# Attention and two mixture layers on one core: operands laid out as the engines read them, and three attention blocks in other slots

## The reference, cut to what matters

```python
scores = scale * np.matmul(q, k.transpose(0, 1, 3, 2))
mask = (rel >= 0) & (rel < 64)            # rel = query position - key position
scores = np.where(mask, scores, -1000000000.0)
attn = softmax(scores)                    # exp(s - max) / (sum + 1e-9)
x = matmul(attn, v)                       # -> (2304, 512), heads side by side
```

## Time and profile before

| | us |
|---|---|
| median of three runs | 1084.02 (1082.53 to 1084.6) |
| the profiled execution, its own time | 1084.5 |
| its span, first to last instruction | 1082.8 |
| TensorE busy | 1047.7 (97%) |
| start of `gate_val(0)`, from the span's start | 40.81 |

### The profile page before, as it was taken

One profiled execution on the slowest core, in us unless ns is written; L12 is line 12 of the kernel. 1 busy time (PEld: TensorE's weight loads), 2 busy tenths in 40 slices (PEclk: granted clock), 3 DMA queues, 4 the chain that ended last, 5 costly groups with the idle time before them and its releaser, 6 DMA issues. The chain is left out here.

```text
span 1082.8 us, 19239 instructions
## 1 busy us (share of the span) xinstructions
PE 1047.7 (97%) x7599; PEld 957.4 (88%) x7599; DVE 404.4 (37%) x1131; ACT 396.5 (37%) x959; POOL 233.9 (22%) x225
## 2 busy tenths in 40 slices
PE   6799999999999999999999999999999999999994
PEld 5699999999999999999999989889898989898993
DVE  4364334343343434333245534423242434342410
ACT  5344343343434334343324532433332433333310
POOL 2266003012021211202012041330403031211211
PEclk8699999999999999999999999999999999999997
DMA  7565214222122222211212350562536354453302
GB/s 160 129 185 118 49 30 108 54 70 60 47 62 50 69 50 79 54 36 31 78 41 89 117 143 30 156 139 85 137 97 152 102 136 117 102 151 90 66 12 38
DMA packets 121211, 95.31 MB, mean 88 GB/s; under 512 B 83232, under 2 KB 95776, under 8 KB 121120
## 3 DMA queue, kind: packets, MB, share of 16 engines
q1 hardware_dynamic: 108032, 66.48, 21.6%
q0 software_dynamic: 12032, 27.31, 12.1%
q10 hardware_dynamic: 1056, 0.26, 0.1%
HBM read 72.35 MB, written 21.68 MB: 87 GB/s over the span
## 5 line engine op out<-in xcount | busy, mean ns | idle before, releaser
L784 PEld LDWEIGHTS bank<-xr,wr 128*128 128x128 f32 x2592 | 326.5, 191 | 9.3 <-issue 0.5
L784 PE MATMUL bank<-xr,wr 128*128 128x256 f32 x2592 | 329.4, 284 | 0.0
L865 PE MATMUL bank<-wr 128*128 128x256 f32 (+1 forms) x1536 | 229.8, 309 | 0.6 <-DVE xr L1439 0.3
L865 PEld LDWEIGHTS bank<-wr 128*128 128x128 f32 x1536 | 226.1, 190 | 1.4 <-DVE wr L1439 0.6
L801 PE MATMUL bank<-wr,hr 128*128 128x512 f32 x648 | 176.4, 407 | 0.0
L1066 ACT ACTIVATE arena<-bank 128x256 f32<-128x256 f32 x108 | 41.3, 383 | 282.6 <-PE bank L784 282.6
L1333 DVE SCALAR_TENSOR_TENSOR arena<-arena,bank 128x256 f32<-128x256 f32 x108 | 45.5, 421 | 259.4 <-ACT arena L1066 252.2
L880 PE MATMUL bank<-wr 128*128 128x512 f32 x576 | 136.3, 393 | 0.0
L801 PEld LDWEIGHTS bank<-wr,hr 128*128 128x128 f32 x648 | 113.7, 189 | 22.9 <-issue 2.8
L880 PEld LDWEIGHTS bank<-wr 128*128 128x128 f32 x576 | 106.6, 188 | 21.5
L602 POOL DMA_INDIRECT out<-arena,tab x34 | 53.4, 1572 | 283.8 <-ACT arena L1145 275.4
(11 more groups left out here) (127 smaller groups left out, 846.6 us busy)
## 6 DMA issues: line engine op xcount, KB each, us to landing
arena<-moe_w SPq DMA_DIRECT2D x64, 512.0 KB, 3.8
arena<-v SPq DMA_DIRECT2D x70, 128.0 KB, 3.2
out<-zeros POOLq DMA_DIRECT2D x20, 256.0 KB, 2.7
arena<-k SPq DMA_DIRECT2D x36, 128.0 KB, 3.1
x_rows<-arena SPq DMA_DIRECT2D x9, 512.0 KB, 2.8
arena<-q SPq DMA_DIRECT2D x34, 128.0 KB, 3.2
arena<-moe_w_gate SPq DMA_DIRECT2D x12, 256.0 KB, 3.3
arena<-moe_w_val SPq DMA_DIRECT2D x12, 256.0 KB, 4.0
```

The lines of the kernel that those rows point to most:

```text
L784: mm = pe.matmul(o, gv_w[:, f, w, kk], xr[:, g % 2, x, kk], start=(m + kk + n == 0), stop=(kk == KC - 1 and n == 2), skip_group_check=True)
L865: mm = pe.matmul(ps_h[u % 2][:, 0:n], w1_r[e % 2][:, a, kk, f * P:(f + 1) * P], xT[p][:, b, kk], start=(kk + x == 0), stop=(kk == KC - 1 a ...
```

## The change

In `kernel`, numpy rearranges four inputs before the launch. q and k become arrays of 18 pairs x 128 x 2 blocks x 4 x 64: 128 partitions hold the head dimension of two heads, so that they land in `qT` and `kT` as the matmul reads them, 2 KB for each partition. v becomes rows of 512 floats. w_gate and w_val become one array `gv`, 4 KB for each partition and chunk. `turn_k`, `turn_q`, `copy_k` and `copy_q` go, with the waits on `q_copied`. `qT` gets two buffers. The factor -1/8 moves into the `scale` of the instruction in `mask_max` (`scale=-SCALE`), and the mask's fill becomes negative. The loads of k and q of pair t now stand in slot 6t-21 and wait for the scores that read the buffer. The scores of block 5 move from the opening into slot 0, turn_p of block 4 into slot 1, and each step of blocks 4 to 7 gets a slot from a table; blocks 8 and on stay in their slots. `split_high` and `split_low` of chunks 0 and 1 stand later in the opening's order.

```diff
+    S_LATE = {5: 0, 6: 2, 7: 4}
+    E_LATE = {5: 1, 6: 3, 7: 5}
+    SUM_LATE = {4: 0, 5: 2, 6: 4, 7: 6}
+    P_LATE = {4: 1, 5: 3, 6: 5, 7: 7}
+    PV_LATE = {4: 2, 5: 4, 6: 6, 7: 8}
+    X_LATE = {4: 3, 5: 5, 6: 7, 7: 10}
+    MIXED_LATE = {3: 3, 7: 4}
+    V_LATE = 5
...
+        def stage(s, offset, late):
+            for n, at in late.items():
+                if at == s:
+                    return n
+            n, off = divmod(s - offset, 3)
+            return n if off == 0 and max(late) < n < NB else None
...
             def load_k(t):
-                if t:
-                    sp.wait_ge(k_turned, t)
-                for half in range(2):
-                    sp.dma_start(k_nat[half * WIN:(half + 1) * WIN].rearrange("p (h d) -> p h d", h=H),
-                                 of_block(k, 2 * t + half)).then_inc(k_in, 16)
+                if t >= 2:
+                    sp.wait_ge(s_done, 2 * t - 1)
+                sp.dma_start(kT[:, t % 2:t % 2 + 3:2], k[t]).then_inc(k_in[t % 2], 16)
             def load_q(t):
-                sp.wait_ge(q_turned, t)
-                for half in range(2):
-                    sp.dma_start(q_nat[half * WIN:(half + 1) * WIN].rearrange("p (h d) -> p h d", h=H),
-                                 of_block(q, 2 * t + half)).then_inc(q_in, 16)
+                if t >= 2:
+                    sp.wait_ge(s_done, 2 * t - 2)
+                sp.dma_start(qT[:, t % 2], q[t]).then_inc(q_in[t % 2], 16)
...
-                for m, src in enumerate((gate_d, val_d)):
-                    sp.dma_start(gv_raw[:, f % 2, m], src[f]).then_inc(gv_in[f % 2], 16)
+                sp.dma_start(gv_raw[:, f % 2].rearrange("p m k n -> p (m k n)"), gv[f]).then_inc(gv_in[f % 2], 16)
...
-            load_k(0)
+            sp.dma_start(kT[:, 0], k[0, :, 0]).then_inc(k_first, 16)
+            sp.dma_start(kT[:, 2], k[0, :, 1]).then_inc(k_in[0], 16)
             load_mixed(0)
             load_v(0)
+            load_k(1)
             load_weights(0)
-            load_k(1)
-            load_q(1)
             load_weights(1)
+            load_k(2)
+            load_q(2)
             load_mixed(1)
-            load_k(2)
             load_v(1)
-            load_q(2)
             load_weights(2)
             load_mixed(2)
+            load_v(2)
             load_k(3)
+            load_q(3)
             load_weights(3)
-            load_v(2)
-            load_q(3)
-            load_k(4)
...
-            turn_k(0)
-            turn_q(0)
             scores(0)
             scores(1)
-            turn_k(1)
-            turn_q(1)
             turn_p(0)
             scores(2)
             values(0)
             turn_p(1)
             scores(3)
             values(1)
             turn_p(2)
-            turn_k(2)
             values(2)
-            turn_q(2)
             turn_p(3)
             values(3)
             scores(4)
-            turn_k(3)
-            turn_q(3)
-            scores(5)
             for s in range(LAST):
                 g, f = divmod(s, FC)
                 if 0 <= s < LAST:
                     gate_val(g, f)
-                if s == 0:
-                    turn_p(OPEN)
-                    values(OPEN)
-                if (n := at_slot(s, 3, -18, NB)) is not None:
+                if (n := stage(s, -18, S_LATE)) is not None:
                     scores(n)
-                if (n := at_slot(s, 3, -14, NB)) is not None:
+                if (n := stage(s, -14, P_LATE)) is not None:
                     turn_p(n)
-                if (n := at_slot(s, 3, -13, NB)) is not None:
+                if (n := stage(s, -13, PV_LATE)) is not None:
                     values(n)
                 if g >= 2 and f == 0:
                     rank_rows(g - 2)
-                if (t := at_slot(s, 6, -20, TT)) is not None:
-                    turn_k(t)
-                if (t := at_slot(s, 6, -19, TT)) is not None:
-                    turn_q(t)
...
-            act.dma_start(q_nat[half * WIN:(half + 1) * WIN].rearrange("p (h d) -> p h d", h=H),
-                              of_block(q, half)).then_inc(q_in, 16)
+            act.dma_start(qT[:, 0, 0], q[0, :, 0]).then_inc(q_first, 16)
+            act.dma_start(qT[:, 0, 1], q[0, :, 1]).then_inc(q_in[0], 16)
+            act.dma_start(qT[:, 1], q[1]).then_inc(q_in[1], 16)
```

More of the change, by code:

```diff
@@ L14, with attention_two_moe_program @@
 P = 128
[L17 to L26, removed]
+def attention_two_moe_program(nc, q, k, v, gv, w_out, r_gate, r_noise, noise, w1, w2, out):
+    TT, P_, _, GP, WIN = q.shape
+    TOK, DM = v.shape
+    HD = P_ // 2
+    FC = gv.shape[0]
+    DF = FC * P
+    NB = 2 * TT
+    B = 4
+    BLOCKS = NB // B
     SCALE = float(HD) ** -0.5
@@ L29, in attention_two_moe_program @@
     KC = DM // P
-    FC = DF // P
     GT = 2 * P
@@ L62, in attention_two_moe_program @@
     assert (CH * TOK + AHEAD * HT - 2 * TILES * P) // P < MORE
-    assert (HD, WIN, GP, KC, FC) == (64, 64, 4, 4, 12) and S == BLOCKS * WIN and NB == 4 * GROUPS == 2 * TT
+    assert (HD, WIN, GP, KC, FC) == (64, 64, 4, 4, 12) and TOK == NB * WIN and NB == 4 * GROUPS == B * BLOCKS
     assert NW == FC * DM
@@ L217, in attention_two_moe_program @@
         out_t = out.rearrange("(t p) d -> t p d", p=P)
-        k_in = sem("k_in")
-        q_in = sem("q_in")
+        k_first = sem("k_first")
+        q_first = sem("q_first")
+        k_in = [sem(f"k_in{u}") for u in range(2)]
+        q_in = [sem(f"q_in{u}") for u in range(2)]
         v_in = sem("v_in")
         m_in = sem("m_in")
[L222 to L225, removed]
         s_done = sem("s_done")
@@ L397, in load_v @@
                     sp.wait_ge(pv_done, 2 * t)
-                for half in range(2):
-                    sp.dma_start(v_nat[half * WIN:(half + 1) * WIN].rearrange("p (h d) -> p h d", h=H),
-                                 of_block(v, 2 * t + half)).then_inc(v_in, 16)
+                sp.dma_start(v_nat[:], v[t * P:(t + 1) * P]).then_inc(v_in, 16)
             def load_mixed(t):
@@ L606, in _ @@
             split_out(1)
-            scale(OPEN)
             for s in range(LAST):
-                if (n := at_slot(s, 3, -15, NB)) is not None:
+                if (n := stage(s, -15, SUM_LATE)) is not None:
                     scale(n)
@@ L679, in _ @@
         def _(pe):
[L680 to L704, removed]
             def scores(n):
                 c0, c1 = keys(n)
-                pe.wait_ge(k_copied, n // 2 + 1)
-                pe.wait_ge(q_copied, n // 2 + 1)
+                if n == 0:
+                    pe.wait_ge(k_first, 16)
+                    pe.wait_ge(q_first, 16)
+                else:
+                    pe.wait_ge(k_in[n // 2 % 2], 16 * (n // 4 + 1))
+                    pe.wait_ge(q_in[n // 2 % 2], 16 * (n // 4 + 1))
                 if n > OPEN:
@@ L725, in scores @@
                             if starts(n):
-                                window = kT[rows, c, place(n)]
+                                window = kT[rows, place(n), c * WIN:(c + 1) * WIN]
                             else:
                                 even, odd = sorted((place(n - 1), place(n)))
-                                window = kT[rows, c, even:odd + 1:odd - even]
-                            mm = pe.matmul(ps_sc(n)[h][j * WIN:(j + 1) * WIN, i * P + c0:i * P + c1], qT[rows, c, n % 2], window,
+                                window = kT[rows, even:odd + 1:odd - even, c * WIN:(c + 1) * WIN]
+                            mm = pe.matmul(ps_sc(n)[h][j * WIN:(j + 1) * WIN, i * P + c0:i * P + c1], qT[rows, n // 2 % 2, n % 2, c * WIN:(c + 1) * WIN], window,
                                            start=True, stop=True)
@@ L1157, in _ @@
             x_high(1)
-            split_high(1)
             copy_pT(2)
-            copy_k(2)
+            split_high(0)
             x_high(2)
@@ L1163, in _ @@
             x_high(3)
+            split_high(1)
             exps(4)
-            copy_k(3)
             for s in range(LAST):
@@ L1170, in _ @@
                     h_high(s)
-                if s == 0:
-                    copy_pT(OPEN)
-                    exps(OPEN + 1)
-                if (n := at_slot(s, 3, -14, NB)) is not None:
+                if (n := stage(s, -14, P_LATE)) is not None:
                     copy_pT(n)
-                if (n := at_slot(s, 3, -11, NB)) is not None:
+                if (n := stage(s, -11, X_LATE)) is not None:
                     x_high(n)
-                if (t := at_slot(s, 6, -20, TT)) is not None:
-                    copy_k(t)
                 if 1 <= g < GROUPS - 1 and f in (2, 3):
@@ L1199, in _ @@
                     high(0, KC + 2 * (s - (LAST - 2)) + 1)
-                if (n := at_slot(s, 3, -16, NB)) is not None:
+                if (n := stage(s, -16, E_LATE)) is not None:
                     exps(n)
@@ L1440, in hidden_low @@
                                          in1=hT[p][:, 0, f].bitcast(F32), op0=ALU.max, op1=ALU.subtract).then_inc(ht_lo, 1)
-            copy_q(0)
```

(29 more changed lines are left out.)

59 lines of the change are left out of this document (17 added, 42 removed).

## The result

The changed kernel takes 1056.46 us (median of four runs, 1055.68 to 1058.44), the kernel before 1084.31 us (1082.53 to 1084.74) beside it. The ratio is 0.9744, with a 95% interval of 0.9732 to 0.9757: 27.9 us less, where 28.6 were forecast. The profiled execution is the longest of the four, 1058.44 us with a span of 1056.8.

What follows compares the result with a forecast made beforehand. TensorE was taken to bound the slots and a chain of small steps the opening. 11.8 + 15.9 + 1.5 - 0.6 = 28.6 us off 1084.5 gives 1055.9, or 1055.5 for the median; range 1051 to 1061.

Steps and rivals of the forecast that it cites:

- What bounds the kernel: Whole kernel: TensorE, busy 1047.7 of 1082.8 us, bounds the slots; a chain of small steps on three engines bounds the opening.
- Part 1: Slots 4 to 83: no turning of q and k for 14 pairs, 0.84 us each, 11.8 us off.
- The strides of `kT` and `qT`: Scores in the slots: no gain seen from other strides; 10% on 36 blocks would be 2.4 us.
- Part 2: Opening: the chain in its new order starts gate_val(0) at 24.9 instead of 40.81 us, 15.9 us off.
- Part 3: Blocks moved among opening and first slots: 1.5 us wait for copy_pT(4) off, scores(5) in slot 0 0.6 us on.
- compressed block: Blocks 4 to 7 in the early slots: stalls priced at 0, with 0.5 us for each block as bad bound.
- The cover of the loads: k and q from pair 4 on: buffer free six slots, some 30 us, before use against 4.7 us landing; no wait.
- A: Opening: a load binds again and costs up to 5.4 us, giving 1061 us; chance 0.12.
- B: Opening and gate_val(0): TensorE's clock rises sooner, 4.7 us less, giving 1051 us; chance 0.15.
- the rule on transposes: TensorE's clock in the opening: transposes do not count as busy time, so removing turning raises the share that counts; unsized.
- C: Slots: TensorE is not what they wait for once turning is gone; 11.8 us not gained, 1067 us; chance 0.02.
- D: Slots: k and q late for scores, over 2.0 us wait in each of 14 pairs, at least 1087 us; chance 0.01.

Runs made afterwards that it cites:

- the second profile: Profile from timing the changed kernel again with nothing altered: 1056.58 us, ratio 0.9738 to the kernel before; the profiled execution took 1054.71 us.
- the fillers: Matmuls on zeros put into the five gaps where TensorE waits in the opening, against the changed kernel: 1051.6 us, 5.0 us less.

## Why the prediction was right, point by point

**What bounds the kernel.** Right. TensorE's pitch set the slots and a chain of short steps the opening; both halves gave time, by different means.

**Part 1, the turning in the slots: 11.8 us.** Right. Putting the transposes back costs 11.3 to 11.6 us by the medians and 11.7 to 12.0 in the profiles, and the slots left have the pitches named, 4.70 and 5.07. The strides of `kT` and `qT` cost nothing: 16 matmuls of scores take 0.67 us, with a pitch of 0.60, after the change too.

**Part 2, the opening: 15.9 us, measured 14.1.** The chain went through the steps named, down to values(1) held by x_low(0) behind mask_max(3). One term of the sum was mis-sized: the step from turn_p(0) to turn_p(1), put at 3.61 us, took 14.65 - 9.80 = 4.85. I had it at full clock (0.44 and 0.87); it ran at half, 0.96 and 1.34, after an idle gap of 2.74 us, 1.0 us more; and scale_first(1) took 1.35 instead of 1.10 beside GpSimd. The step from turn_p(1) to values(1) was put 0.3 us too short (3.77, measured 4.05); the others are right to about 0.1. In the second profile of the same kernel the step from turn_p(0) to turn_p(1) took 3.34 us, with the clock up and a scale_first(1) of 0.74, and gate_val(0) came at 24.33. The forecast of 24.9 lies between the two. The term is off by what the clock and scale_first(1) do from run to run, so that the medians agree to 1 us owes something to luck. What the opening gained without the move, 40.81 - 29.44 = 11.4 us, comes from the turning, the order of the loads and the order on ScalarE and VectorE together; no run tells these apart.

**Part 3, the moved blocks: 0.9 us net.** The wait of 1.50 us went and scores(5) came in at 0.60, as forecast. What I had put wholly down to the opening belongs here in part: the move is worth 4.8 us with the new layout, and 6.6 us alone. The layout without the move gives 1061.4, 23.7 us less than before. The sum is not touched by this, since what the move gave stood in part 2. No compressed block stalled: TensorE has no gap from 31 us until the experts' stage.

**The cover of the loads.** Right: a lead of one slot is enough, a lead of none costs 82.8 us.

**The rivals.** A is out (small pieces move nothing, no load is in the list of waits). B did not come by itself: the clock was at 0.50 from 24 to 30 us though the turning was gone, so its removal was not enough. What spoke for B, a TensorE busy in some 80% of 17 to 25 us, came true in the second profile (6.5 of 8 us) and not in the first (4.8 of 8), and the clock was at 0.50 there in both. The window of before that was to bear out the rule on transposes held three sets of transposes, but only two of them were turning; the third was a turn_p. No run tests that rule apart. B's price was about right, 4.7 us against the 5.0 that the fillers gave. C is out by the transposes put back. D needed the lead gone.

## What to carry to other kernels

Price an instruction on the bounding engine by the pitch between its neighbours with and without it; here that gave 11.8 us for 11.3 to 12.0. In a chain of short steps ask of each step which clock the gap ahead of it leaves, and what is queued behind what on the engines that are not the bound: moving a block out of the opening uncovered an x_low behind a mask_max. Where TensorE must wait in short gaps, independent matmuls in them can pay, but only as many as end before the wait does.

## What the runs showed of the hardware that was not expected

A wait of 3.7 to 4.3 us on TensorE in dense slots costs another 2.4 us through the clock, since scores, out_rows and part of the next gate_val behind it run at 1.2 GHz. In the opening, where waits of 2.7, 1.9, 1.9, 0.8 and 0.8 us stand between short bursts, the clock is at 0.50 from 10 us on, and filling them holds it at 1.00. The moment at which the clock rises during the warming differs between executions of one program (3.86 or 4.61 us for the same twenty records), and so does the moment at which it falls. The first moved gate_val(0) by 0.7 us and the second by 0.9, of 2.35 between two profiles.

The same VectorE instruction, scale_first(1), takes 0.70 to 1.73 us in the profiles of the changed kernel and its variants, while GpSimd works beside it; those of blocks 2 and 3, when GpSimd is idle, take 0.69 us. No run was made to test this.
